# Attention probabilities transposed in 32x32 blocks on VectorE and put in order by DMA, in place of TensorE transposes, in an attention + two-MLP kernel

## The reference

```python
# q, k, v: (4 batches, 8 heads, 576 positions, 64)
# attention within chunks of 64 positions, per batch, head and chunk:
scores = q_c @ k_c.T / 8
attn = exp(scores - max(scores)); attn = attn / (sum(attn) + 1e-9)
x = concat_heads(attn @ v_c)                      # 2304 tokens x 512
h = x @ w_in;   x = (h - tanh(h)) @ w_out         # first MLP, 512 -> 2048 -> 512
h = x @ w_in2;  out = (h * tanh(softplus(h))) @ w_out2   # second MLP
```

## Time and profile before

| | |
|---|---|
| median of 3 runs | 832.12 us |
| the profiled execution: its own time, its span | 832.69 us, 830.9 us |
| PE busy | 814.8 us, 98% of the span |
| DVE busy | 536.0 us, 65% |
| ACT busy | 372.0 us, 45% |
| POOL busy | 151.4 us, 18% |
| four transposes a turn, 18 turns (L807) | 72 matmuls, 15 of the turns lie within the first MLP |
| DMA | 128.27 MB, mean 154 GB/s |

### The profile page before, as it was taken

The page is one execution under the profiler, slowest core; times in us unless marked ns, Lnnn a source line. Parts: engine busy times, 40 slices in busy tenths (PEclk is TensorE's granted clock), DMA queues, the critical chain, the costliest instruction groups (busy, mean ns, idle before and its releaser), DMA issues.

```text
span 830.9 us, 13448 instructions
## 1 busy us (share of the span) xinstructions
PE 814.8 (98%) x5400; PEld 766.5 (92%) x5400; DVE 536.0 (65%) x806; ACT 372.0 (45%) x586; POOL 151.4 (18%) x212
## 2 busy tenths in 40 slices
PE   4999999999999999999999999999999999999997
PEld 3999999999999999999999988888888888988996
DVE  5766655545555464534446788888877777877775
ACT  4554444444344444334335445546445445535434
POOL 4221344334404423310110021110000000000000
PEclk9999999999999999999999999999999999999999
DMA  7542254415514432521655255488424366523302
GB/s 253 179 165 78 76 191 159 147 77 190 186 69 153 162 119 107 187 77 67 224 178 203 89 177 196 172 306 318 185 89 149 118 243 246 207 90 124 142 1 76
DMA packets 35837, 128.27 MB, mean 154 GB/s; under 512 B 5184, under 2 KB 5184, under 8 KB 35776
## 3 DMA queue, kind: packets, MB, share of 16 engines
q1 hardware_dynamic: 23328, 79.44, 26.3%
q0 software_dynamic: 12448, 47.98, 16.3%
HBM read 91.49 MB, written 35.91 MB: 153 GB/s over the span
## 4 chain that ended last, share of the span: by engine, by line
PE 91%; DVE 5%; ACT 2%; DMA 1%; issue 1%; SPq 0%; DVEq 0%; ACTq 0%
PE psum L862 8%; PE psum L864 8%; PE psum L863 8%; PE psum L849 8%; PE psum L850 8%; PE psum L851 8%; PE psum L985 7%; PE psum L986 7%; PE psum L984 7%; PE psum L963 6%; PE psum L964 6%; PE psum L962 6%; PE psum L824 1%; PE psum L807 1%; PE psum L795 1%; DMA pool_words<-kT 1%
## 5 line engine op out<-in xcount | busy, mean ns | idle before, releaser
L615 DVE TENSOR_TENSOR pool_words<-psum,pool_words 128x384 f32<-128x384 f32 x96 | 53.5, 557 | 139.8 <-ACT pool_words L427 139.8
L864 PE MATMUL psum<-g_hi,w_lo 128*128 128x384 f32 x384 | 128.4, 334 | 0.0
L862 PE MATMUL psum<-g_hi,w_hi 128*128 128x384 f32 x384 | 128.3, 334 | 0.0
L863 PE MATMUL psum<-g_lo,w_hi 128*128 128x384 f32 x384 | 128.3, 334 | 0.0
L849 PE MATMUL psum<-x_hi,w_hi 128*128 128x384 f32 x360 | 123.4, 343 | 0.0
L850 PE MATMUL psum<-x_lo,w_hi 128*128 128x384 f32 x360 | 120.3, 334 | 0.0
L851 PE MATMUL psum<-x_hi,w_lo 128*128 128x384 f32 x360 | 120.3, 334 | 0.0
L427 ACT ACTIVATE pool_words<-psum 128x384 f32<-128x384 f32 x96 | 46.8, 488 | 129.6 <-PE psum L851 126.9
L963 PE MATMUL psum<-w_lo,w_hi 128*128 128x384 f32 x288 | 97.5, 338 | 0.0
L964 PE MATMUL psum<-w_hi,w_lo 128*128 128x384 f32 x288 | 97.0, 337 | 0.0
L962 PE MATMUL psum<-w_hi 128*128 128x384 f32 x288 | 96.3, 334 | 0.0
(11 more groups left out here) (101 smaller groups left out, 1540.4 us busy)
## 6 DMA issues: line engine op xcount, KB each, us to landing
w_hi<-s_hi SPq DMA_DIRECT2D x24, 896.0 KB, 4.6
w_lo<-s_lo SPq DMA_DIRECT2D x24, 896.0 KB, 6.4
pool_words<-w_out POOLq DMA_DIRECT2D x32, 256.0 KB, 3.8
w_hi<-t_hi SPq DMA_DIRECT2D x18, 384.0 KB, 5.2
w_lo<-t_lo SPq DMA_DIRECT2D x18, 384.0 KB, 6.2
pool_words<-w POOLq DMA_DIRECT2D x24, 256.0 KB, 3.7
pool_words<-qT SPq DMA_DIRECT2D x18, 256.0 KB, 3.5
pool_words<-kT SPq DMA_DIRECT2D x18, 256.0 KB, 4.6
```

Of the source, the lines that this page charges most:

```text
L862: pe.matmul(ps, w_hi[:, 1, cols], g_hi[:, s, :], start=f == 0, stop=False)
L863: pe.matmul(ps, w_hi[:, 1, cols], g_lo[:, s, :], start=False, stop=False)
L864: mm = pe.matmul(ps, w_lo[:, 1, cols], g_hi[:, s, :], start=False, stop=f == FT - 1)
```

## The change

Tiles 3 to 17 (those whose attention lies within the first MLP) no longer use `turn` and `copy_turned`. Behind `normalise(t)`, VectorE transposes the probabilities of the tile in one instruction, `turn_blocks(t)`: every block of 32x32 by itself. What is left is to exchange blocks between groups of 32 partitions: SP issues eight DMAs for it (`order_blocks(t)`), each of 32 partitions and 256 words, from SBUF to SBUF, back into the words of the probabilities. `values(t)` waits for all eight, and reads v in another order of rows, which the host lays out. Tiles 0 to 2 stay as they were.

The blocks of `values(t)` and `scores(t + 1)` are at f = 6, 10, 14 in group 0, and at f = 4, 9, 14 in groups 1 to 4. The preparing step of f = 5 goes to f = 6.

```diff
-TURN_AT = {3 + 4 * i: i for i in range(GROUP_TILES)}
-BLOCK_AT = {5 + 4 * i: i for i in range(GROUP_TILES)}
+def block_at(g):
+    if g == GROUPS - 1:
+        return {}
+    return {f: i for i, f in enumerate((6, 10, 14) if g == 0 else (4, 9, 14))}
-SLOTS = (2, 3, 4, 5, 7, 8, 9, 11, 12, 13)
+SLOTS = (2, 3, 4, 6, 7, 8, 9, 11, 12, 13)
+        turned_blocks = region[:, 4 * words:5 * words].rearrange("p (a h q) -> p a h q", a=2, h=HEADS)
+        ordered_words = region[:, 3 * words:4 * words]
+        v_by_chunk = region[:, 2 * words:3 * words].rearrange("p (m r e d) -> p m r e d", m=2, r=2, e=2)
 # SP
+            def order_blocks(t):
+                sp.wait_ge(blocks_turned, t - GROUP_TILES + 1)
+                for c in range(2):
+                    for q1 in range(2):
+                        for k1 in range(2):
+                            rows, to_rows = (slice(c * CHUNK + 32 * h, c * CHUNK + 32 * h + 32) for h in (q1, k1))
+                            sp.dma_start(ordered_words[to_rows, q1 * 256:(q1 + 1) * 256],
+                                         turned_blocks[rows, k1, :, :].rearrange("p h q -> p (h q)")).then_inc(blocks_ordered, 16)
             for t in range(GROUP_TILES, TILES):
                 sp.wait_ge(scores_ready, t)
                 load_qk(t)
+                if t > GROUP_TILES:
+                    order_blocks(t - 1)
                 sp.wait_ge(values_ready, t)
                 load_v(t)
+            order_blocks(TILES - 1)
 # VectorE
+            def turn_blocks(t):
+                dve.wait_ge(probs_ready, t + 1)
+                if t == GROUP_TILES:
+                    dve.wait_ge(values_ready, GROUP_TILES)
+                dve.transpose(turned_blocks, ordered_words.rearrange("p (h a k) -> p a h k", h=HEADS, a=2)).then_inc(blocks_turned, 1)
                     if scores_of is not None:
                         normalise(scores_of)
+                        turn_blocks(scores_of)
 # TensorE
             def wait_for_values(t):
-                pe.wait_ge(turned_copied, t + 1)
+                if t < GROUP_TILES:
+                    pe.wait_ge(turned_copied, t + 1)
+                else:
+                    pe.wait_ge(blocks_ordered, 128 * (t - GROUP_TILES + 1))
             def values(t):
+                if t >= GROUP_TILES:
+                    ordered = ordered_words.rearrange("p (a h q) -> p h a q", a=2, h=HEADS)
+                    for m in range(2):
+                        for r in range(2):
+                            for c, e in QUARTERS:
+                                mm = pe.matmul(ps[half(e), c, (2 * m + r) * CHUNK:(2 * m + r + 1) * CHUNK], v_by_chunk[half(c), m, r, e, :],
+                                               ordered[half(c), 4 * m + 2 * e + r, :, :], start=True, stop=True)
+                    mm.then_inc(values_ready, 1)
+                    return
-                    if not last and f in TURN_AT:
-                        turn(t0 + TURN_AT[f])
```

More of the change, by code:

```diff
@@ L202, in build @@
         norm_steps, probs_ready = sem("norm_steps"), sem("probs_ready")
+        blocks_turned, blocks_ordered = sem("blocks_turned"), sem("blocks_ordered")
         turned, turned_copied, values_ready, x_next_done = sem("turned"), sem("turned_copied"), sem("values_ready"), sem("x_next_done")
@@ L412, in keep_x @@
                     act.wait_ge(x_lo_done, KT * splits)
-                act.activation(x_next[:, :, i * P:(i + 1) * P].rearrange("p (m r) s -> p r m s", m=2),
-                               attention_banks(t)[1].rearrange("p r (m s) -> p r m s", m=2), ACT.Copy).then_inc(x_next_done, 1)
+                to = x_next[:, :, i * P:(i + 1) * P]
+                if t < GROUP_TILES:
+                    act.activation(to.rearrange("p (m r) s -> p r m s", m=2),
+                                   attention_banks(t)[1].rearrange("p r (m s) -> p r m s", m=2), ACT.Copy).then_inc(x_next_done, 1)
+                else:
+                    act.activation(to.rearrange("p k (c s) -> p c k s", c=2),
+                                   attention_banks(t)[1].rearrange("p c (k s) -> p c k s", k=KT), ACT.Copy).then_inc(x_next_done, 1)
             def split_x_hi(g):
@@ L466, in mlp1_group @@
                         exps(t0)
[L467 to L471, removed]
+                    if f - 1 in block_at(g):
+                        t = t0 + block_at(g)[f - 1]
+                        keep_x(t, block_at(g)[f - 1], g + 1)
                         if t + 1 < TILES:
@@ L588, in shift @@
                 dve.wait_ge(max_done, t + 1)
-                if t >= 2:
+                if 2 <= t <= GROUP_TILES:
                     dve.wait_ge(turned, (t - 1) if t == 2 else t)
+                if t > GROUP_TILES:
+                    dve.wait_ge(values_ready, t)
                 dve.tensor_tensor(probs, scores, row_max[:, :, :].unsqueeze(3).broadcast_to((P, 2, 4, CHUNK)),
@@ L645, in mlp1_group @@
                         scores_of = t0
-                    if not last and f - 1 in BLOCK_AT and t0 + BLOCK_AT[f - 1] + 1 < TILES:
-                        scores_of = t0 + BLOCK_AT[f - 1] + 1
+                    if f - 1 in block_at(g) and t0 + block_at(g)[f - 1] + 1 < TILES:
+                        scores_of = t0 + block_at(g)[f - 1] + 1
                     if scores_of is not None:
@@ L818, in values @@
             def values(t):
+                ps = attention_banks(t)[1]
+                if t >= GROUP_TILES:
[7 more added lines that the diff above has]
+                    return
                 _, _, v_sb, _, probs_t = views_of(t)
-                ps = attention_banks(t)[1]
                 for m in range(2):
@@ L874, in mlp1_group @@
                         wait_for_scores(t0)
[L875 to L878, removed]
+                    if f in block_at(g):
+                        wait_for_values(t0 + block_at(g)[f])
+                        if t0 + block_at(g)[f] + 1 < TILES:
+                            wait_for_scores(t0 + block_at(g)[f] + 1)
                     if f >= lag:
@@ L884, in mlp1_group @@
                         scores(t0)
-                    if not last and f in TURN_AT:
-                        turn(t0 + TURN_AT[f])
[L887 to L890, removed]
+                    if f in block_at(g):
+                        values(t0 + block_at(g)[f])
+                        if t0 + block_at(g)[f] + 1 < TILES:
+                            scores(t0 + block_at(g)[f] + 1)
                 if not last:
@@ L1028 @@
         "kT": np.ascontiguousarray(by_tile(k).transpose(0, 2, 6, 4, 3, 1, 5)).reshape(TILES, P, HEADS * CHUNK),
-        "v": np.ascontiguousarray(by_tile(v).transpose(0, 3, 5, 2, 4, 1, 6)).reshape(TILES, P, HEADS * CHUNK),
+        "v": np.concatenate([by_tile(v)[:GROUP_TILES].transpose(0, 3, 5, 2, 4, 1, 6).reshape(GROUP_TILES, P, HEADS * CHUNK),
+                             by_tile(v)[GROUP_TILES:].transpose(0, 1, 5, 2, 3, 4, 6).reshape(TILES - GROUP_TILES, P, HEADS * CHUNK)]),
         "w1": np.ascontiguousarray(moe_w_in), "w1_out": np.ascontiguousarray(moe_w_out),
```

2 lines of the change are left out of this document (removed).

## The result

The changed kernel takes 827.49 us in the median of 6 runs (825.29 to 828.95), the kernel before, run beside it, 832.35 us (831.77 to 835.15). These two medians are 4.9 us apart; the recorded ratio is 0.9929, with a 95% interval from 0.9916 to 0.9943, which is 5.9 us faster (4.7 to 7.0). A second series of five runs gave 0.9914 (0.9901 to 0.9928). I had forecast 825.7 us from 832.1, 6.4 less.

The account below looks back on a forecast made before the run. TensorE was taken as the bound, busy 98% of the span. From 832.69 us profiled, - 6.6 for turns and + 0.2 at group 0's seam gave 826.3, or 825.7 us for the runs; range 824.6 to 829.0.

Parts of the forecast that it names:

- The turns: TensorE's transposes in the first MLP: a turn costs 0.44 us, so 15 changed tiles give back 6.6 us.
- rival 5: A transpose holds TensorE for its whole duration: 1.09 us a turn, 16.3 us in all, 816 us; 2%.
- The blocks and the split read: Moved blocks, values reading two runs of 32 words: no change taken, ends -0.8 and +7.7 us in all.
- Rival 4: The values matmuls suffer from the split read: up to +7.7 us, 833.4 us; 4%.
- The block transpose: On VectorE behind the softmax: 0.7 us a tile, hidden, with g_lo behind it 3 us to spare.
- The DMAs: SP's eight issues a tile, 0.33 to 0.43 us each: tile in order at 12.3 us, all 15 in time.
- Rival 2: Part shows, tiles 4 and 5 ordered late or g_lo at group 0's seam: together 3.2 us, 829 us; 12%.
- The seam: Third block's softmax falls into step 15: no wait at ordinary seams, a loss of 0.2 us at group 0's.
- The sum: Profiled execution 832.69 us - 6.6 + 0.2 = 826.3; the runs should show 825.7 us.
- Rival 1: Everything on the other engines and queues is hidden: 825.7 us (824.6 to 826.8); 74%.
- my own sign: TensorE waiting for the ordering DMAs in group 0 alone would show case 2 right; in groups 1 to 4, case 3.
- Rival 3: SP's small transfers go one behind another or issue slowly: tiles late by 49 us together, 875 us; 8%.

Follow-up runs that it names:

- e1: The kernel before with the turns and their copies of tiles 3 to 17 left out and nothing in their place; 828.04 us, ratio 0.9932.
- e5: The changed kernel with the weights' split of step 2 in group 0 ahead of tile 3's block transpose on VectorE; 827.00 us, ratio to before 0.9924.
- e7: The changed kernel with the weights' split ahead of tile 3's block transpose and group 0's order wait behind y1; 826.11 us, ratio to before 0.9912.
- e2: The kernel before, TensorE transposes kept, with only the blocks moved to the new positions and each turn two steps ahead; 833.34 us, ratio 0.9998.
- e3: The changed kernel without the eight ordering DMAs of each tile, values reading the block transpose's result as it is; 827.25 us, ratio to before 0.9917.
- e6: The changed kernel with TensorE's wait for a tile's order behind y1 instead of ahead, group 0 only; 827.19 us, ratio to before 0.9922.
- e4: The changed kernel with each ordering DMA cut into two of 128 words, 16 a tile; 845.03 us, ratio to before 1.0132.

## Why the prediction was right, point by point

**The turns, right.** 0.44 us from the earlier trace rows was 0.447 in the steady groups, and the 12 turns of groups 1 to 4 are 5.4 of the 6.0 us won there. Reading the distance between starts and not the duration made the difference to rival 5.

**The blocks and the split read, right.** I took no change and it is none; e1 and the changed kernel agree to 0.01 us in a group. Rival 4 falls. (The profile counts 32 rows for the 16 matmuls of the values in the kernel's text, and 32 for those of the scores, before as after.)

**The block transpose: the size right, the cover wrong at one place.** It takes 0.711 us where I took 0.7. I followed what stands behind it on VectorE only to `g_lo`. In group 0 the split of the weights stands ahead of that, and `hidden` waits for it two steps later. The split ends at 36.88 with the transpose, so at 36.17 without it, and TensorE asks for it at 36.09. Before, the turn of step 3 stood ahead of that `hidden` and gave it 0.44 us more. Both the missing turn and the transpose eat up this cover, and 0.9 us were lost: 0.7 by the transpose (e5, e7) and 0.2 by the missing turn (e1, e2). Had I named what is queued behind the transpose in group 0 too, this term would have been in the sum.

**The DMAs: the issue mis-sized, the outcome half foreseen.** An issue takes 0.59 us and not up to 0.43, so a tile is in order not at 12.3 but at 6.4 + 5.0 + 1.9 = 13.3 us with the median landing, and tile 4, with its slow last landing, at 15.4. The margin of the nine tiles at 18.7 us was ample. Rival 2 named tile 4 with 0.1 us in hand at the slow end, and 0.9 us were lost (e3, e6). Its 3.2 us were too much. The 2.0 us that the prediction takes there from the Trainium skill (DMA: Bandwidth & Descriptors, Anatomy of one DMA) are given there for DMAs that GpSimd issues. SP's pieces landed after 1.9 us in the median.

**The seam: right for groups 1 to 4, wrong in sign for group 0.** I charged 0.2 us there, since POOL's sums would keep their place against `hidden(0, 15)`. They moved forward, and 0.6 us were won (e2).

**The sum.** -6.7 (turns) - 0.6 (first seam) + 0.9 (w_lo) + 0.9 (tile 4) is -5.5 us, and with the 0.6 us behind the last store, which no term of mine had, -6.1; the measured gain is 4.7 to 7.0. My -6.4 lies there too, but partly by luck: two gains that I had not foreseen, 0.6 at the seam and 0.6 at the end, cover most of the two losses of 0.9. Rival 1, everything hidden and at most 826.8 us, is not what happened: by my own sign, waits in group 0 alone, it is rival 2 in a milder form, which I had given 12%. The time itself, 827.49, is 1.8 above the forecast. Some 0.3 of that is the sum. The other 1.5 us are in the profiled execution the later start of group 0 (0.20) and the slower way to `scores(3)` (1.26), so that the spans close: 830.9 - 6.1 + 1.5 = 826.3. The start has nothing to do with the change, and other executions of the kernel before fit it: the three runs that I started from took 831.8 to 832.2, and the 35 runs of the same kernel beside the experiments 833.6 in the median.

**Rival 3.** Its mechanism is real, as e4 shows, with a price for each piece on SP's queue. I had put the turning point at 17.9 us behind the hidden step and charged a late tile with its wait alone. With waits of 3.8 us the clock falls as well, so it may lie earlier where one wait grows that long; a wait of 3.3 us, as I had it there, was not measured.

## What to carry to other kernels

Where TensorE is the bound, price its small instructions by the distance between the starts of their neighbours, and move them away if the other engines' queues have room. For everything added to another engine's queue, list what stands behind it in every kind of step, the steps of the first group with their own work too, and compare each with the time at which TensorE asks for it, which comes earlier once something is taken out of TensorE's own queue. Ordering data by small DMAs costs by the piece, so it can be hidden behind a long enough wait, and if it is not long enough, TensorE's clock may add to the price: 3.8 us of waiting cost 6.7.

## What the runs showed that I had not expected

- The end of the span, behind the issue of the last store, is 0.6 us shorter in all eight profiles with ordering DMAs than in the four without (2.5 against 3.1 us). The cause is open.
- A DMA from SBUF to SBUF of 32 partitions takes SP 0.59 us to issue, with 256 words a partition as with 128, while one of 128 partitions and 512 words from memory takes 0.43 or less. It lands sooner, after 1.9 us.
- The granted-clock record says 1.00 for the first matmuls of group 0 while their starts are 0.32 us apart, and 0.50 for the same distance behind e4's wait. So at the start of a program I trust the distance; no run separates the two.
- Without POOL beside it, the four x_lo instructions at the first seam take 1.96 us, with it 3.60, and POOL's sum 0.73 against 1.05: both lose.
